# Sums of features on GpSimd in halves, a reordered unit of attention, another order of features, and a last product taken bank by bank

## What is computed

```python
# q, k, v: (4, 8, 576, 64) float32; factor = 4
out_d = softmax(scale * q_d @ k_d.T) @ v_d          # q_d, k_d, v_d: means over 4 rows, 144 of them
out_up = repeat(out_d, 4, axis=2)
out_local = softmax(where(abs(i - j) < 4, scale * q @ k.T, -1e9)) @ v
x = (out_up + out_local) as (2304, 512)
x = silu(x @ w_in) @ w_out                          # 512 -> 2048 -> 512
y = g(x @ w2_in) @ w2_out, g(h) = h / (1 + exp(-1.702 h))
```

## Time and profile before

| | |
|---|---|
| median of three runs | 829.08 us (828.62 to 831.41) |
| the profiled execution's own time | 831.32 us |
| its span, first to last instruction | 829.4 us |
| mean granted TensorE clock | 0.994 |
| TensorE, VectorE, ScalarE, GpSimd busy | 97%, 79%, 65%, 23% |
| attention, until TensorE's first matmul of the products | 113.83 us |
| last second stage begins, last VectorE instruction begins | 767.16 us, 825.61 us |

### The profile page before, as it was taken

How to read it: one execution, slowest core, us unless ns; L and a number is a source line. 1 busy time by engine, 2 the same in 40 slices (tenths; PEclk the granted TensorE clock), 3 DMA queues, 4 the chain that set the end, 5 groups by cost and what they waited for, 6 DMA issues and landing times.

```text
span 829.4 us, 15638 instructions
## 1 busy us (share of the span) xinstructions
PE 806.5 (97%) x5787; PEld 778.4 (94%) x5787; DVE 653.4 (79%) x945; ACT 536.2 (65%) x865; POOL 191.8 (23%) x191
## 2 busy tenths in 40 slices
PE   7988899999999999999999999999999999999998
PEld 4766679999999999999999999999999999999997
DVE  6889869989989867888767888899756677665465
ACT  5887775667735567745677555687465787365763
POOL 6678768612025511036300000000000000000000
PEclk8999999999999999999999999999999999999999
DMA  7878756877677897768887787877887777878773
GB/s 211 246 196 231 200 163 234 276 245 260 205 247 249 274 311 263 251 209 262 265 288 254 232 258 251 271 244 235 301 282 260 265 252 265 290 241 267 270 260 126
DMA packets 98315, 205.42 MB, mean 248 GB/s; under 512 B 8416, under 2 KB 56032, under 8 KB 98240
## 3 DMA queue, kind: packets, MB, share of 16 engines
q1 hardware_dynamic: 98240, 204.42, 75.5%
HBM read 160.87 MB, written 43.52 MB: 246 GB/s over the span
## 4 chain that ended last, share of the span: by engine, by line
PE 76%; DVE 8%; DMA 6%; issue 3%; POOL 3%; ACT 2%; SPq 0%; DVEq 0%; POOLq 0%; ACTq 0%
PE hid L322 39%; PE yp L345 35%; DMA vn<-in_v 5%; DVE gr L498 2%; POOL vpair L897 2%; DMA wr<-in_w_in 1%; DVE wh L294 1%; DVE xs L255 1%; PE pt L1090 1%; ACT xs L251 1%; ACT wh L285 0%; DVE x L1063 0%; ACT yt L938 0%; POOL pband L900 0%; ACT pavg L988 0%
## 5 line engine op out<-in xcount | busy, mean ns | idle before, releaser
L322 PE MATMUL hid<-xs,wh 128*128 128x384 f32 x2016 | 352.9, 335 | 3.2 <-DVE hw L478 2.1
L322 PEld LDWEIGHTS hid<-xs,wh 128*128 128x128 f32 x2016 | 349.0, 188 | 6.1 <-issue 4.8
L345 PE MATMUL yp<-gr,wh 128*128 128x384 f32 x2016 | 352.5, 335 | 1.8 <-DVE gr L498 1.8
L345 PEld LDWEIGHTS yp<-gr,wh 128*128 128x128 f32 x2016 | 351.0, 189 | 2.3 <-issue 2.3
L285 ACT ACTIVATE wh<-wr 128x1024 fp32r<-128x1024 f32 (+1 forms) x164 | 164.5, 1003 | 157.7 <-PE hid L322 118.0
L498 DVE TENSOR_TENSOR gr<-G,gr 128x768 fp32r<-128x768 f32 x144 | 138.6, 971 | 48.3 <-ACT gr L398 48.2
L398 ACT ACTIVATE gr<-G 128x768 fp32r<-128x768 f32 x144 | 121.8, 846 | 68.9 <-PE yp L345 67.6
L294 DVE TENSOR_TENSOR wh<-wr,wh 128x1024 fp32r<-128x1024 f32 x76 | 89.4, 1176 | 23.1 <-ACT wh L285 23.0
L365 ACT ACTIVATE G<-G 128x1152 f32<-128x1152 f32 x48 | 55.8, 1162 | 0.0
L488 DVE TENSOR_TENSOR G<-hv,hid 128x384 f32<-128x384 f32 x48 | 26.5, 552 | 27.0 <-PE hid L322 26.9
L473 DVE TENSOR_TENSOR hv<-p,hid 128x384 f32<-128x384 f32 x48 | 26.4, 549 | 26.9 <-PE hid L322 19.3
(11 more groups left out here) (94 smaller groups left out, 766.8 us busy)
## 6 DMA issues: line engine op xcount, KB each, us to landing
wh<-rests SPq DMA_DIRECT2D x72, 512.0 KB, 3.8
wr<-sums_out SPq DMA_DIRECT2D x48, 512.0 KB, 4.7
wr<-in_w_out SPq DMA_DIRECT2D x36, 512.0 KB, 5.2
rests<-wh SPq DMA_DIRECT2D x36, 512.0 KB, 3.3
wr<-sums_in SPq DMA_DIRECT2D x40, 384.0 KB, 4.0
wr<-in_w_in SPq DMA_DIRECT2D x40, 256.0 KB, 3.4
qk<-in_qkT SPq DMA_DIRECT2D x11, 576.0 KB, 6.3
G<-in_w_in SPq DMA_DIRECT2D x12, 512.0 KB, 7.2
```

Of the source, the lines that this page charges most:

```text
L322: last = eng.matmul(hid[:, at, 0:HALF], lhsT=wh[:, w % SLOTS, part, a % 4, cc * P:(cc + 1) * P], rhs=xs[:, rest, q, cc, :], start=start an ...
L345: last = eng.matmul(yp[:, at + m, 0:HALF], lhsT=wh[:, w % SLOTS, part, p % 4, m * P:(m + 1) * P], rhs=gr[:, p, rest, :], start=start and p ...
```

## The change

- **FILLS**: the features of the next block are prepared in the order B11, B21, T1, B22, T3, T2, T4. The sums T1, T3, T2, T4 follow at steps 0, 1, 2 and 3 (before: two at step 0, then 1 and 4).
- **First block**: `sum_x` gets a `chunk`; GpSimd makes each of the four sums in two halves of 128x384, one in each of units 7 to 14, after its sums of weights. VectorE makes none. Roundings go to units 3, 5, 9, 10, 11, 13 and 15, of weights to 4, 6 and 7, rests to the unit behind each. The roundings wait for the x of the unit before (at most for eight units' x).
- **GpSimd's unit**: `pband` first, then `vpair`, `vavg` (two buffers) and the sums of weights of pair (n - 1) // 2, none in unit 0, all four in unit 15.
- **SyncE's unit**: q and k first, then v_half and vn, then vwin, and in even units the raw weights.
- **Start**: the filling matmuls use `zeros`, cleared by VectorE; seven more come after unit 0's coarse scores, six after unit 1's scores. GpSimd makes the band masks before the identity.
- **Second stages**: `results(n)` and ScalarE's rounding come first in step 6. In blocks 0 and 3 three of the four t2 sums are made in the first stage (pairs 2, 4 and 6) and one at step 1; the four t4 sums at steps 2 and 3.
- **Last product**: all pairs for the first bank, then all for the second; each bank is added and stored by itself.

```diff
-FILLS = (B11, T1, T3, T2, B21, B22, T4)
+FILLS = (B11, B21, T1, B22, T3, T2, T4)
...
                 eng.wait_ge(self.x_lo, 7 * n + FILLS.index({T1: B11, T2: T1, T4: B21}[q]) + 1)
-            eng.tensor_tensor(features(n, q), a, b, ALU.subtract).then_inc(self.x_sum, 1)
+            if chunk is None:
+                eng.tensor_tensor(features(n, q), a, b, ALU.subtract).then_inc(self.x_sum, 1)
+            else:
+                eng.tensor_tensor(features(n, q)[:, chunk], a[:, chunk], b[:, chunk], ALU.subtract).then_inc(
+                    self.x_sum if chunk else self.x_half, 1)
+                if not chunk:
+                    eng.wait_ge(self.x_half, XSUM[q])
         def prepare_x(eng, n, i):
...
             rest_x(eng, n, FILLS[i])
-            for q in {B11: (T1, T3), T1: (T2,), B21: (T4,)}.get(FILLS[i], ()):
+            for q in {B11: (T1,), B21: (T3,), T1: (T2,), B22: (T4,)}.get(FILLS[i], ()):
...
         def round_weights(eng, w):
...
                     eng.wait_ge(self.y_copy, 5 * n + i - 1)
+                if n == N - 1 and i == 6:
+                    last_product(w=BATCHES * n + 28)
+                    return
...
+            def last_product(w):
+                for m in range(2):
+                    for p in range(PAIRS):
+                        if m == 0 and p % 4 == 0:
+                            split(eng, w + p // 4)
+                        if m == 0 and p % 2 == 0:
+                            eng.wait_ge(self.g_lo, 24 * (N - 1) + 20 + p // 2 + 1)
+                        for j, (part, rest) in enumerate(((0, 0), (0, 1), (1, 0))):
+                            last = eng.matmul(
+                                yp[:, m, 0:HALF], lhsT=wh[:, (w + p // 4) % SLOTS, part, p % 4, m * P:(m + 1) * P],
+                                rhs=gr[:, p, rest, :], start=False, stop=p == 7 and j == 2, skip_group_check=True)
+                    last.then_inc(self.bank, 1)
...
                     gate_rest(PAIRS * n + 7, self.GATE[layer_of(n)])
+                if i == 6:
+                    round_x(eng, n + 1, FILLS[i])
...
                         round_weights(eng, w + SLOTS)
-                    if a == 2:
+                    if a == 2 and i < 6:
...
                 eng.tensor_tensor(G[:, p, G22, :], hw[:], hid[:, 3, 0:HALF], ALU.add).then_inc(self.h_sum, 1)
+                if n in EARLY_T2 and p in (2, 4, 6):
+                    sum_t2(n, p // 2 - 1)
...
                     sum_t3(PAIRS * n + 7)
+                if i == 6:
+                    results(n)
...
                         rest_weights(eng, w + SLOTS)
-                        if 2 <= i < 4:
+                        if n in EARLY_T2:
+                            if 2 <= i < 4:
+                                sum_t4(n, 2 * i - 4)
+                        elif 2 <= i < 4:
...
                     if a == 3:
-                        if 2 <= i < 4:
+                        if n in EARLY_T2:
+                            if i == 1:
+                                sum_t2(n, 3)
+                            elif 2 <= i < 4:
+                                sum_t4(n, 2 * i - 3)
+                        elif 2 <= i < 4:
...
                                 sum_t4(n, b)
-                if i == 6:
-                    results(n)
...
                     second(n, i)
-            last_result(N - 1)
+            for m in range(2):
+                eng.wait_ge(self.bank, m + 1)
+                eng.scalar_tensor_tensor(quarter(N - 1, 1, 0)[:, m], yp[:, m, 0:HALF], 1.0 / self.GATE[1], yt[:, 0, m],
+                                         ALU.mult, ALU.add).then_inc(self.y_last, 1)
         def gpsimd(eng):
...
                     store(n, 1, 1, (self.y_sum, 5 * n + 4))
-            store(N - 1, 1, 0, (self.y_sum, 5 * N))
-            eng.wait_ge(self.y_out, 4 * DMA_INC * self.BLOCKS)
+            for m in range(2):
+                at = (N - 1) % self.BLOCKS * self.TOKENS
+                eng.wait_ge(self.y_last, m + 1)
+                eng.dma_start(self.out[:, 2 + m, at:at + HALF], quarter(N - 1, 1, 0)[:, m]).then_inc(
+                    self.y_out, DMA_INC)
+            eng.wait_ge(self.y_out, (4 * self.BLOCKS + 1) * DMA_INC)
...
+    ROUNDED = (3, 5, 9, 10, 11, 13, 15)
+    ROUNDED_W = (4, 6, 7)
+    SUMMED = {7: (T1, 0), 8: (T1, 1), 9: (T3, 0), 10: (T3, 1), 11: (T2, 0), 12: (T2, 1), 13: (T4, 0), 14: (T4, 1)}
...
+    IDLE = (7, 6)
...
             def body(u, first=False):
-                if u.n + 1 < UNITS:
-                    eng.wait_ge(v_half, u.n + 1)
-                    load_vn(u.after())
...
                 if u.n + 1 < UNITS:
+                    eng.wait_ge(v_half, u.n + 1)
+                    load_vn(u.after())
...
                         load_vwin(u.after())
-                if u.odd and u.n + 1 < UNITS:
-                    eng.wait_ge(ffn.w0_sum, 2 * u.n)
-                    ffn.first_raw(eng, u.half + 1)
+                if not u.odd:
+                    if u.half:
+                        eng.wait_ge(ffn.w0_sum, 4 * u.half - 2)
+                    ffn.first_raw(eng, u.half)
             start(Unit(0, 0))
-            ffn.first_raw(eng, 0)
...
             eng.sem_inc(consts, 1)
+            identity(ident16)
+            eng.wait_ge(consts, 2)
...
+                eng.wait_ge(b_rcp, u.n + 1)
+                e = pband[u.odd]
+                eng.tensor_tensor(e[:, :, 0:WIN], e[:, :, 0:WIN], rcb[:].unsqueeze(2).broadcast_to([P, NT, WIN]),
+                                  ALU.mult).then_inc(b_nrm, 1)
...
                 eng.tensor_tensor(vpair[:], rows[:, 0:2], rows[:, 2:4], ALU.add).then_inc(v_half, 1)
-                eng.wait_ge(b_rcp, u.n + 1)
-                e = pband[u.odd]
-                eng.tensor_tensor(e[:, :, 0:WIN], e[:, :, 0:WIN], rcb[:].unsqueeze(2).broadcast_to([P, NT, WIN]),
-                                  ALU.mult).then_inc(b_nrm, 1)
                 eng.wait_ge(v_half, u.n + 1)
+                if u.n > 1:
+                    eng.wait_ge(avg_out, u.n - 1)
+                eng.tensor_tensor(vavg[u.odd][0:HP], vpair[:, 0], vpair[:, 1], ALU.add).then_inc(v_sum, 1)
                 if not first:
-                    eng.wait_ge(avg_out, u.n)
-                eng.tensor_tensor(vavg[0:HP], vpair[:, 0], vpair[:, 1], ALU.add).then_inc(v_sum, 1)
-                sum_weights(u)
+                    sum_weights(u)
+                if u.n in SUMMED:
+                    eng.wait_ge(x_done, 1 + min(u.n - 1, 8))
+                    ffn.sum_x(eng, 0, *SUMMED[u.n])
             def sum_weights(u):
+                p = (u.n - 1) // 2
                 def at(a):
-                    return ffn.first_place(u.half, a)
+                    return ffn.first_place(p, a)
                 if u.odd:
-                    eng.wait_ge(ffn.w0_sum, 2 * u.n)
-                    eng.tensor_tensor(at(S2), at(S1), at(A11), ALU.subtract).then_inc(ffn.w0_sum, 1)
-                    eng.wait_ge(ffn.w0_sum, 2 * u.n + 1)
-                    eng.tensor_tensor(at(S4), at(A12), at(S2), ALU.subtract).then_inc(ffn.w0_sum, 1)
-                else:
-                    eng.wait_ge(ffn.w0_in, DMA_INC * (u.half + 1))
+                    eng.wait_ge(ffn.w0_in, DMA_INC * (p + 1))
...
                     eng.tensor_tensor(at(S3), at(A11), at(A21), ALU.subtract).then_inc(ffn.w0_sum, 1)
+                if not u.odd or u.n + 1 == UNITS:
+                    eng.wait_ge(ffn.w0_sum, 4 * p + 2)
+                    eng.tensor_tensor(at(S2), at(S1), at(A11), ALU.subtract).then_inc(ffn.w0_sum, 1)
+                    eng.wait_ge(ffn.w0_sum, 4 * p + 3)
+                    eng.tensor_tensor(at(S4), at(A12), at(S2), ALU.subtract).then_inc(ffn.w0_sum, 1)
...
                 eng.wait_ge(pads_too, n + 1)
-            eng.wait_ge(pads, 5)
+            eng.wait_ge(pads, 6)
...
             def early(n):
-                if n in (3, 4, 5):
-                    ffn.round_weights(eng, n - 3)
-                elif n == 6:
-                    eng.wait_ge(x_done, 1 + 2)
-                    ffn.round_x(eng, 0, B11)
-                elif 8 <= n < 14:
-                    eng.wait_ge(x_done, 1 + n)
-                    ffn.round_x(eng, 0, FILLS[n - 7])
-            eng.wait_ge(consts, 2)
+                if n in ROUNDED_W:
+                    ffn.round_weights(eng, ROUNDED_W.index(n))
+                elif n in ROUNDED:
+                    eng.wait_ge(x_done, 1 + min(n - 1, 8))
+                    ffn.round_x(eng, 0, FILLS[ROUNDED.index(n)])
+            eng.wait_ge(consts, 1)
...
             def early(n):
-                if n in (4, 5, 6):
-                    ffn.rest_weights(eng, n - 4)
-                elif n in (8, 13):
-                    ffn.sum_x(eng, 0, T1 if n == 8 else T4)
-                elif n in (9, 10):
-                    ffn.sum_x(eng, 0, T3 if n == 9 else T2)
-                if n in (7, 9, 10, 11, 12, 14, 15):
-                    ffn.rest_x(eng, 0, FILLS[(7, 9, 10, 11, 12, 14, 15).index(n)])
```

(23 more changed lines are left out.)

16 lines of the change are left out of this document (9 added, 7 removed).

## The result

The changed kernel takes 818.79 us, the median of six runs (816.29 to 820.69), beside 828.80 for the kernel before in the same comparison (827.47 to 831.41). The ratio is 0.9877, with a 95% interval of 0.9853 to 0.9901: 1.2% faster. The forecast was 812.6 with a range to 819.0, so the direction and the kind of gain came as foretold. The size was 10.0 us instead of 16.5, and the time lies 0.2 us inside the end of the range. The profiled execution has a span of 816.5 us and a time of 818.3 us.

The account below looks back on a forecast made before the run. TensorE, busy 97% of the span, was taken as the bound, so only its stands and half-clock time counted. Terms -2.5 - 6.9 - 6.4 - 0.7 = -16.5 gave 814.8 profiled, 812.6 as median; range 807.5 to 819.0.

Parts of the forecast that it names:

- signs of being wrong: Attention and products: a unit from 7 on above 7 us, pband long after rcb, or product stages stretching at t2 sums.
- the GpSimd rival: Attention units 7 to 14: GpSimd becomes the bound, eight units take 7.1 us, +5.6 us, 818.2; chance 0.13.
- Start, -2.5: Start of the attention: filling matmuls keep TensorE's clock at 2.4 GHz; -2.5 us, between 0 and -3.2.
- Order on GpSimd and SyncE: Attention units: pband's multiply precedes vpair, so a late vn no longer holds TensorE's transposes; counted within the units' -6.9 us.
- The first block's features, -6.9 for the units: Attention units: four sums leave VectorE for GpSimd as eight halves; 4.1 of 10.96 us lost stay, -6.9, between 0 and -10.
- with misses of vn and raw weights I allow 3.0 us in all: Attention units: allowance of 3.0 us for GpSimd's lateness, including late fetches, within the 4.1 us expected to stay.
- The port: Attention units 7 to 14: four VectorE rests each wait for a GpSimd half, +4.0 us, 816.6; chance 0.05.
- The clock: Start of the attention: rival that the clock falls all the same, start returns only 0.3 us, 814.8; chance 0.07.
- Products, -6.4: Product stages: reordered feature sums and earlier results(n) end TensorE's waits; -6.4 us, between +0.5 and -7.8.
- Last product, -0.7: End of the kernel: finishing bank by bank shortens the last addition and halves the last store; -0.7 us, between 0 and -1.
- From the profiled time to the median: Whole kernel: median taken as 2.2 us below the profiled time, as in the kernel before; 814.8 became 812.6.

Follow-up runs that it names:

- no_fill: The changed kernel without the seven and six filling matmuls behind the scores of units 0 and 1: 819.39 us, ratio 0.9896 to the kernel before.
- sums_vector: The changed kernel with the first block's four feature sums back on VectorE, whole, in units 9, 11, 13 and 15: 814.81 us, ratio 0.9839.
- the two loads: sums_vector with a useless GpSimd instruction of about 1 us in units 7 to 14: a fill, 819.16 us, or a subtraction reading two operands, 818.58 us.
- results_late: The changed kernel with results(n) behind the rest of step 6 again, ScalarE's rounding of T4 staying early: 819.76 us, ratio 0.9880.

## Why the prediction was right, and where it was off

The forecast of 812.6 was not met: 818.79 lies 0.2 us inside the range, and the repetition, 817.80, 1.2 us inside. That the range held is in part luck. Its upper end takes in two rivals, and the time that came about is near that of the GpSimd rival, 818.2, which had a chance of 0.13. Two of the prediction's own signs of being wrong appeared in the trace: units from 7 on that exceed 7 us (9.30 and 7.24), and a pband that starts long after rcb (89.71 after 88.37). The third, stretched product stages, did not.

- *Start, -2.5:* right, 2.26 by the trace, and 1.6 of it by the fills, as no_fill showed.
- *Order on GpSimd and SyncE:* no gain of it is shown. "A late vn no longer holds the transposes" is true of the profile, but with the old order in place the kernel is as fast, and TensorE waits for pband no less than before the change (5.4 us against 4.6). The step took the recorded waits as losses that the new order would end. That the old order pays for them by releasing vn earlier is argued, not shown. The order was tried only together with the halves; without them, in sums_vector, the waits for pband are 1.8 us, and what the old order would make of that was not run.
- *The first block's features, -6.9 for the units:* the mechanism was named and mis-sized. A half costs 1.00 us, as I took it; the waits of TensorE for ScalarE's work are gone, which no run ascribes to one of the edits, though with the sums back on VectorE they stay away. The term that failed is "with misses of vn and raw weights I allow 3.0 us in all". TensorE alone waits 5.4 us for pband, and the units keep 7.84 us above the floor instead of 4.1, with the halves about 3 us of it, as sums_vector and the two loads show. I had compared GpSimd's work with the unit's length on average, 5.6 and 6.5 with 6.1. (Its terms add up to 4.67, not 4.6, and the units without a sum are six of the fourteen, not of sixteen; neither matters.) But the start of pband is not free in the unit: it must come between rcb and the transposes, and a fully loaded engine misses that by whatever was late before it. The rival in which GpSimd becomes the bound is the one that came about, at 3.7 of its 5.6 us.
- *The port:* VectorE was held, as the rival had it: 2.62 us instead of 1.22. It was held in one rest and not in four (the feature rests there took 0.94 to 1.09), and the fill of the same length costs as much as the read, so the collision is there and not the cause. The Trainium skill, SBUF — State Buffer, section "SBUF: two separate sides", says that the one of the two which starts first has the pair for the whole instruction. The trace agrees in that one stands while the other runs, and does not in every case by the order of the recorded starts: in results_late GpSimd's sum of weights began at 58.33 and lasted 2.12 us, while VectorE's rest began after it, at 58.65, and kept its 1.22:

```profile
58.33 2.12 POOL L977 TENSOR_TENSOR G<-G 128x256 f32<-128x256 f32 x1 [0.49 <-DMA G<-in_w_in]
...
58.65 1.22 DVE L301 TENSOR_TENSOR wh<-G,wh 128x1024 fp32r<-128x1024 f32 x1
```

- *The clock:* foreseen for the start alone. That a late pband in the middle can bring it down, at 1.75 us of standing, was in no step. Unit 9 took 9.30 us with the fall, and 7.53 to 7.83 in the five traces with the halves and the new order in which the clock did not fall there.
- *Products, -6.4:* right in the sum, 6.58. Early t2 and t4 are worth 2.4 us, results(n) 1.4 by the trace and nothing clear by the medians; the third part, in the last block, has lost its explanation.
- *Last product, -0.7:* right, 0.7 to 1.0.
- *From the profiled time to the median:* I carried the 2.2 us by which the profiled execution of the kernel before was slower than its median over to the changed kernel. That was wrong: it lies within the scatter of single executions. Other executions of the kernel before took 827.3 to 832.4 us, and the changed kernel's profiled time, 818.3, is 0.5 below its median. So about 2.5 us of the 12.9 read off the traces belong to one slow execution of the kernel before, and can't be placed in a term. The forecast of 814.8 for the profiled time missed by 3.5 us, the one for the median by 6.2.

## What to carry to other kernels

An engine off the critical path that takes over work must be judged by its latest start in each round, not by its share: here 1 us more on GpSimd in eight rounds that had on average room for it cost about 3 us, through an instruction queued behind it. Give such work to the engine that has slack at the right moment; the sums on VectorE, spread over four units, made the fastest kernel of this study (814.8 us, 0.9839). And a fetch moved earlier is only worth something if the fetch that it then meets had slack.
